# Attention over channels and two gated MLPs on one core: the head rearranged (first loads on two queues, seven split segments, sums of squares folded in PSUM, another TensorE order)

## What is computed

```python
qn = q / (norm(q, axis=1) + 1e-6)          # q, k, v: (1, 6016, 256)
kn = k / (norm(k, axis=1) + 1e-6)
a = softmax(kn.transpose(0, 2, 1) @ qn / tau, axis=-1)   # 256 x 256
x = (v @ a).reshape(6016, 256)
x = (silu(x @ w_gate) * (x @ w_val)) @ w_out             # 256 -> 1536 -> 256
h = x @ w_in                                             # 256 -> 2048
out = (h * clip(h + 3, 0, 6) / 6) @ w_out2               # -> 256
```

## Time and profile before

| | |
|---|---|
| median of 3 runs (lowest, highest) | 1163.73 us (1163.48, 1164.4) |
| the profiled execution: its time, its span | 1163.87 us, 1162.0 us |
| TensorE busy | 1151.7 us, 99% of the span |
| TensorE granted clock, mean | 0.999 |
| VectorE, ScalarE, GpSimd busy | 61%, 23%, 6% |
| first matmul of the main loop; its second | 67.73 us; 68.56 us |

### The profile page before, as it was taken

How to read it: one execution, slowest core, us unless ns; L and a number is a source line. 1 busy time by engine, 2 the same in 40 slices (tenths; PEclk the granted TensorE clock), 3 DMA queues, 4 the chain that set the end, 5 groups by cost and what they waited for, 6 DMA issues and landing times.

```text
span 1162.0 us, 14581 instructions
## 1 busy us (share of the span) xinstructions
PE 1151.7 (99%) x5212; PEld 967.1 (83%) x5212; DVE 711.5 (61%) x1160; ACT 271.8 (23%) x447; POOL 69.7 (6%) x40
## 2 busy tenths in 40 slices
PE   8999999999999999999999999999999999999998
PEld 7878888888888888888888888888888888888998
DVE  5797764664665574485485476466457557548555
ACT  7731311221221221121121122122122122112121
POOL 5593000000000000000000000000000000000000
PEclk9999999999999999999999999999999999999999
DMA  9642020010002002002002002000100200100100
GB/s 354 234 127 55 1 36 0 0 28 8 0 1 35 0 0 36 0 0 37 0 0 36 0 0 36 0 0 15 21 0 0 36 0 0 32 0 0 19 1 14
DMA packets 108751, 33.76 MB, mean 29 GB/s; under 512 B 98752, under 2 KB 103104, under 8 KB 108736
## 3 DMA queue, kind: packets, MB, share of 16 engines
q1 hardware_dynamic: 106704, 33.10, 11.3%
q10 hardware_dynamic: 2032, 0.46, 0.2%
HBM read 27.39 MB, written 6.16 MB: 29 GB/s over the span
## 4 chain that ended last, share of the span: by engine, by line
PE 96%; DVE 2%; DMA 1%; issue 1%; ACT 0%; SPq 0%; ACTq 0%
PE psum L676 33%; PE psum L699 33%; PE psum L687 22%; PE psum L711 6%; PE psum L584 1%; PE psum L659 1%; DMA qk<-in_k 1%; DVE sq_sum L438 1%; DVE vT L452 0%; DVE sq_sum L444 0%; DVE val_w L511 0%; SPq L252 0%; DVE v_turned L498 0%; PE psum L626 0%; ACT qk_parts L349 0%
## 5 line engine op out<-in xcount | busy, mean ns | idle before, releaser
L699 PE MATMUL psum<-prod,down_w 128*128 128x512 f32 (+1 forms) x1728 | 426.9, 384 | 0.0
L699 PEld LDWEIGHTS psum<-prod,down_w 128*128 128x128 f32 x1728 | 322.6, 188 | 61.7
L687 PE MATMUL psum<-yT,up_w 128*128 128x512 f32 (+1 forms) x1152 | 281.4, 384 | 0.0
L687 PEld LDWEIGHTS psum<-yT,up_w 128*128 128x128 f32 x1152 | 214.9, 188 | 41.3
L540 DVE TENSOR_TENSOR act_out<-psum,act_out 128x512 f32<-128x512 f32 (+1 forms) x144 | 97.9, 680 | 236.3 <-PE psum L676 236.3
L676 PE MATMUL psum<-vT,gate_w 128*128 128x512 f32 (+1 forms) x864 | 215.8, 385 | 0.4 <-DVE vT L452 0.4
L676 PE MATMUL psum<-vT,val_w 128*128 128x512 f32 (+1 forms) x864 | 215.4, 384 | 0.0
L402 ACT ACTIVATE act_out<-psum 128x512 f32<-128x512 f32 (+1 forms) x144 | 85.1, 591 | 471.3 <-PE psum L676 448.3
L676 PEld LDWEIGHTS psum<-vT,gate_w 128*128 128x128 f32 x864 | 161.2, 188 | 32.0 <-DVE vT L452 0.9
L676 PEld LDWEIGHTS psum<-vT,val_w 128*128 128x128 f32 x864 | 161.3, 188 | 30.9
L553 DVE SCALAR_TENSOR_TENSOR act_out<-act_out,psum 128x512 f32<-128x512 f32 (+1 forms) x192 | 129.2, 673 | 76.6 <-ACT act_out L410 76.5
(11 more groups left out here) (66 smaller groups left out, 310.4 us busy)
## 6 DMA issues: line engine op xcount, KB each, us to landing
v_in<-in_v SPq DMA_DIRECT2D x44, 128.0 KB, 3.3
out<-out_sb SPq DMA_DIRECT2D x44, 128.0 KB, 2.5
qk<-in_q SPq DMA_DIRECT2D x7, 512.0 KB, 9.1
qk<-in_k SPq DMA_DIRECT2D x7, 512.0 KB, 10.2
w_stage<-in_moe_w_out SPq DMA_DIRECT2D x7, 512.0 KB, 3.9
w_stage<-in_moe_w_in SPq DMA_DIRECT2D x4, 512.0 KB, 3.8
qk_more<-in_q SPq DMA_DIRECT2D x3, 512.0 KB, 10.5
qk_more<-in_k SPq DMA_DIRECT2D x3, 512.0 KB, 11.2
```

The costliest lines, as they stand in the source:

```text
L687: end = mm(HID[j % 4][:, 0:n], up2_w[:, part, b, j * P:(j + 1) * P], yT[:, m, b, 0:n], start=(part, m, b) == (0, 0, 0), stop=(part, m, b) ...
L699: end = mm(banks[h][:, 0:n], w[:, part, j, h * P:(h + 1) * P], prod[:, c % 4, m, 0:n], start=j == 0 and (part, m) == PASSES[0], stop=False)
```

## The change

It does the following. The loads of k for segment 0 are issued on ScalarE's queue, with q's on SP's; `tau` is issued after the squares of the first chunks. Segment 0 is no longer split; segments 1 to 7 are (seven in place of six), in four buffers (`parts_early`, `parts_late`). ScalarE casts only q's high part; GpSimd casts k's (512 columns) and makes both low parts. The last full segment's squares are added in halves of 512 columns, and the folds of `sq_sum` read or write PSUM; segment 11's squares have a bank of their own. TensorE takes NORMS after segment 9 h = 0, with the rest of the halves behind it, and two chunks and segment 11 of h = 1 behind `turn_exp(0)`. v's first tile is transposed into PSUM banks 0 and 1 ahead of the folds, its evictions stand at folds 2 and 4. The table load for Silu moves behind fold 6; the casts of up blocks 3 and 4 stand ahead of the first exponential, block 5 behind the second.

```diff
-    SPLIT_SEGS = 6
-    WHOLE_SEGS = 9
-    EARLY_CASTS = 3
+    SPLIT = range(1, 8)
+    HALVED = 9
+    FULL_SEGS = SEGS - 1
+    BUFFERS = 4
+    EARLY_CASTS, MIDDLE_CASTS = 3, 2
...
+            parts_late = sb("parts_late", [P, 2, 2, 2, NARROW * C], fp32r, early)
...
+        SQ_BOTH = psum[:, 4:8, :].rearrange("p (h b) c -> p h (b c)", h=2)
+        SQ_LAST = psum[:, 3, :].rearrange("p (h c) -> p h c", h=2)
+        V_FIRST = [psum[:, c, :] for c in range(KC)]
...
+        TURNED = (2, 4)
+
+        def load(queue, s, x, begin, end, loaded):
+            at = seg_at(s)
+            queue.dma_start(slot(s)[:, x, begin:end], (q_seg, k_seg)[x][:, at + begin:at + end]).then_inc(loaded, 16)
...
+        def parts(s):
+            n = SPLIT.index(s) % BUFFERS
+            return parts_early[:, n] if n < 2 else parts_late[:, n - 2]
...
-            def load(s, begin, end, loaded):
-                at = seg_at(s)
-                sp.dma_start(slot(s)[:, 0, begin:end], q_seg[:, at + begin:at + end]).then_inc(loaded, 16)
-                sp.dma_start(slot(s)[:, 1, begin:end], k_seg[:, at + begin:at + end]).then_inc(loaded, 16)
-
-            load(0, 0, WIDE * C, seg_loaded[0])
-            load(0, WIDE * C, SEG * C, narrow_loaded)
-            for s in range(1, SLOTS):
-                load(s, 0, SEG * C, seg_loaded[s])
-            for s in range(SLOTS, SEGS):
-
-                sp.wait_ge(seg_multiplied, s - SLOTS + 1)
-                sp.wait_ge(seg_low, min(s - SLOTS + 1, SPLIT_SEGS))
-                sp.wait_ge(squared, 2 * (s - SLOTS + 1))
-                load(s, 0, seg_chunks(s) * C, seg_loaded[s])
+            load(sp, 0, 0, 0, WIDE * C, seg_loaded[0])
+            load(sp, 0, 0, WIDE * C, SEG * C, rest_loaded)
+
+            for s in range(1, SEGS):
+                if s >= SLOTS:
+
+                    sp.wait_ge(seg_multiplied, s - SLOTS + 1)
+                    if s - SLOTS in SPLIT:
+                        sp.wait_ge(q_high, SPLIT.index(s - SLOTS) + 1)
+                        sp.wait_ge(seg_low, SPLIT.index(s - SLOTS) + 1)
+                    sp.wait_ge(squared, 2 * (s - SLOTS + 1))
+                for x in range(2):
+                    load(sp, s, x, 0, seg_chunks(s) * C, seg_loaded[s])
...
-            for s in range(SPLIT_SEGS):
-                pool.wait_ge(seg_high, s + 1)
-                nc.gpsimd.tensor_tensor(qk_parts[:, s % 2, 1], narrow(s), qk_parts[:, s % 2, 0].bitcast(fp32),
+            for i, s in enumerate(SPLIT):
+                pool.wait_ge(seg_loaded[s], 32)
+                if i >= BUFFERS:
+                    pool.wait_ge(parts_used, i - BUFFERS + 1)
+                nc.gpsimd.tensor_copy(parts(s)[:, 0, 1], narrow(s)[:, 1]).then_inc(k_high, 1)
+                pool.wait_ge(k_high, i + 1)
+                pool.wait_ge(q_high, i + 1)
+                nc.gpsimd.tensor_tensor(parts(s)[:, 1], narrow(s), parts(s)[:, 0].bitcast(fp32),
                                         ALU.subtract).then_inc(seg_low, 1)
...
-            act.dma_start(tau_sb[:, :], tau.to_broadcast([P, 1])).then_inc(tau_loaded, 16)
+            load(act, 0, 1, 0, WIDE * C, seg_loaded[0])
+            load(act, 0, 1, WIDE * C, SEG * C, rest_loaded)
...
+            act.dma_start(tau_sb[:, :], tau.to_broadcast([P, 1])).then_inc(tau_loaded, 16)
+
+            for s in range(FULL_SEGS):
                 act.wait_ge(seg_loaded[s], 32)
                 if s == 0:
-                    act.wait_ge(narrow_loaded, 32)
-                if s < SPLIT_SEGS:
-                    if s >= 2:
-                        act.wait_ge(parts_used, s - 1)
-                    nc.scalar.copy(qk_parts[:, s % 2, 0], narrow(s)).then_inc(seg_high, 1)
+                    act.wait_ge(rest_loaded, 32)
+                if s in SPLIT:
+                    i = SPLIT.index(s)
+                    if i >= BUFFERS:
+                        act.wait_ge(parts_used, i - BUFFERS + 1)
+                    nc.scalar.copy(parts(s)[:, 0, 0], narrow(s)[:, 0]).then_inc(q_high, 1)
                 for h in range(2):
                     if s >= 1:
                         act.wait_ge(squares_added, 2 * (s - 1) + h + 1)
-                    nc.scalar.activation(SQ[h][:, 0:width], slot(s)[:, h, 0:width], ACT.Square).then_inc(squared, 1)
+                    nc.scalar.activation(SQ[h], slot(s)[:, h, :], ACT.Square).then_inc(squared, 1)
+            act.wait_ge(seg_loaded[FULL_SEGS], 32)
+            nc.scalar.activation(SQ_LAST, slot(FULL_SEGS)[:, :, 0:LAST_CHUNKS * C], ACT.Square).then_inc(squared, 1)
...
-            cast_up(EARLY_CASTS)
+            for i in range(EARLY_CASTS, EARLY_CASTS + MIDDLE_CASTS):
+                cast_up(i)
 
             def vT_evict(n, c):
-                act.wait_ge(v_read, n * KC + (c + 1))
-                nc.scalar.copy(vT[:, 0, c, :], v_turned[:, c, :]).then_inc(vT_high, 1)
+                act.wait_ge(v_read, c + 1 if n is None else n * KC + (c + 1))
+                turned = V_FIRST[c] if n is None else v_turned[:, c, :]
+                nc.scalar.copy(vT[:, 0, c, :], turned).then_inc(vT_high, 1)
...
-            cast_up(EARLY_CASTS + 1)
             expT_evict(0)
             exponent(1)
-            cast_up(EARLY_CASTS + 2)
-            table_of(ACT.Silu)
...
-                if r in (6, 8):
-                    vT_evict(0, (6, 8).index(r))
+                if r == 6:
+                    table_of(ACT.Silu)
+                if r in TURNED:
+                    vT_evict(None, TURNED.index(r))
...
-            added = 2 * (SEGS - 1)
-            for width in (2 * C, C):
-                dve.wait_ge(squares_added, added)
-                nc.vector.tensor_tensor(sq_sum[:, :, 0:width], sq_sum[:, :, 0:width], sq_sum[:, :, width:2 * width],
+            added = 2 * (FULL_SEGS - 1)
+            half = 2 * C
+            for h in range(2):
+                dve.wait_ge(squared, 2 * (FULL_SEGS - 1) + h + 1)
+                dve.wait_ge(squares_added, 2 * (FULL_SEGS - 2) + h + 1)
+                nc.vector.tensor_tensor(sq_sum[:, h, 0:half], SQ[h][:, 0:half], sq_sum[:, h, 0:half],
                                         ALU.add).then_inc(squares_added, 1)
-                added += 1
+                nc.vector.tensor_tensor(SQ[h][:, half:], SQ[h][:, half:], sq_sum[:, h, half:],
+                                        ALU.add).then_inc(squares_added, 1)
+            added += 4
             dve.wait_ge(squares_added, added)
-            dve.wait_ge(squared, 2 * SEGS)
-            nc.vector.tensor_tensor(sq_sum[:, :, 0:C], SQ_LAST, sq_sum[:, :, 0:C], ALU.add).then_inc(squares_added, 1)
+            nc.vector.tensor_tensor(sq_sum[:, :, 0:C], SQ_BOTH[:, :, half:half + C], sq_sum[:, :, 0:C],
+                                    ALU.add).then_inc(squares_added, 1)
+            nc.vector.tensor_tensor(SQ_BOTH[:, :, half + C:], SQ_BOTH[:, :, half + C:], sq_sum[:, :, C:half],
+                                    ALU.add).then_inc(squares_added, 1)
+            added += 2
+            dve.wait_ge(squares_added, added)
+            nc.vector.tensor_tensor(sq_sum[:, :, 0:C], SQ_BOTH[:, :, half + C:], sq_sum[:, :, 0:C],
+                                    ALU.add).then_inc(squares_added, 1)
+            added += 1
+            dve.wait_ge(squares_added, added)
+            dve.wait_ge(squared, 2 * FULL_SEGS + 1)
+            nc.vector.tensor_tensor(sq_sum[:, :, 0:C], SQ_LAST, sq_sum[:, :, 0:C],
+                                    ALU.add).then_inc(squares_added, 1)
...
+            for c in range(KC):
+                turn_v(None, c)
...
-                if r in (5, 7):
-                    turn_v(0, (5, 7).index(r))
-                if r in (6, 8):
-                    vT_evict(0, (6, 8).index(r))
+                if r in TURNED:
+                    vT_evict(None, TURNED.index(r))
...
+            wide(0, range(WIDE), range(KC))
+            pe.wait_ge(rest_loaded, 32)
+            wide(0, range(WIDE, SEG), range(KC)).then_inc(seg_multiplied, 1)
+
+            for s in SPLIT:
                 wide(s, range(WIDE), range(KC)).then_inc(seg_multiplied, 1)
-                if s >= 1:
+                if s - 1 in SPLIT:
                     split_part(s - 1)
-            split_part(SPLIT_SEGS - 1)
-            for s in range(SPLIT_SEGS, WHOLE_SEGS):
+            split_part(SPLIT[-1])
+            for s in range(SPLIT.stop, HALVED):
                 wide(s, range(SEG), range(KC))
 
-            for s in range(WHOLE_SEGS, SEGS - 1):
-                wide(s, range(SEG), (0,))
-            pe.wait_ge(squares_added, 2 * (SEGS - 1) + 3)
+
+            wide(HALVED, range(SEG), (0,))
+            pe.wait_ge(squares_added, 2 * (FULL_SEGS - 1) + 8)
             for x in range(2 * KC):
                 end = mm(NORMS[:, x:x + 1], sq_sum[:, x // KC, x % KC * P:(x % KC + 1) * P], ones[:, 0:1],
                          start=True, stop=True)
             end.then_inc(norms_summed, 1)
-            wide(SEGS - 1, range(LAST_CHUNKS), (0,), stop=True).then_inc(scores_summed, 1)
```

(44 more changed lines are left out.)

7 lines of the change are left out of this document (2 added, 5 removed).

## The result

| | before | changed |
|---|---|---|
| median of 13 runs (lowest, highest) | 1164.12 us (1163.48, 1165.21) | 1161.04 us (1160.53, 1166.24) |
| ratio to before, 95% interval | | 0.9978 (0.9969 to 0.9987) |
| profiled execution: time, span | 1163.87, 1162.0 us | 1161.04, 1159.2 us |
| NORMS begins; first fold; second matmul of the main loop | 43.86; 51.02; 68.56 us | 41.43; 48.95; 65.98 us |

The kernel is about 0.2% faster, 2.8 us in the profiled executions, and 2.58 of them stand in the head. From the second matmul of the main loop to the end of the span it is 1093.44 us before and 1093.22 after.

The account below looks back on a forecast made before the run. TensorE is busy 99%, so only the head can give: VectorE's sums decide NORMS. The fold's start gains 1.6 us and vT 0.6, 2.2 in all: 1163.87 to 1161.65, less 0.14 is 1161.5 us; range 1162.3 to 1159.5.

Parts of the forecast that it names:

- The total: Whole kernel: 2.2 us gained in the head, 1.6 by the fold's start and 0.6 by vT, giving 1161.5 us.
- The sums decide: Ahead of NORMS: VectorE's sums end at 41.55 us, TensorE arrives at 39.8 and waits 1.75; loads set the pace.
- rival (b): VectorE's first add waits for late tau; landing at 15 to 17.5 costs 1 to 4 us; chance 0.12 with (d).
- The loads: First loads, 3.5 to 7.0 us: tau causes the 2.05 us loss; issuing it later gains the stream 0.3 us.
- Four buffers: Split segments: casts no longer wait for TensorE's buffers, which spread segments over 3.16 us; adds come every 2.375 to 2.48.
- The tail of the sums: VectorE behind segment 10's add: four half adds and the folds take 5.45 us where it was 5.09.
- From NORMS to the folds: TensorE, NORMS to first fold: 14 matmuls instead of 10, 7.8 us where it was 7.16, no bubble left.
- vT: Start of the main loop: turning v ahead of the folds removes the wait for vT, 0.60 us.
- The covers: Folds: Silu table load, second exponential and casts cost nothing, with over 4 us of cover; about 1 us if it failed.
- Rival (d), the clock: TensorE's clock falls in the wait before NORMS; each microsecond of matmuls would cost one more; chance 0.12 with (b).

Follow-up runs that it names:

- the late wait for tau: Changed kernel with VectorE's wait for tau and its one multiply moved from ahead of the first add to behind the last fold: 1161.04 us, ratio 0.9979.
- the changed kernel's second profile: The changed kernel itself timed again, nothing changed, on one chip with two other runs: median 1160.95 us, ratio 0.9972; the profiled execution took 1162.19 us.

## Why the prediction was right, point by point

**The total.** 1161.5 forecast, 1161.04 measured; second matmul of the loop at 66.34 and at 65.98. The head gained 2.58 us where the sum had 2.22: 0.17 more by the sums, 0.28 more behind NORMS, 0.09 less at vT.

**The sums decide: right in size, wrong in what paces them.** Folds done at 41.55 forecast, 41.38 measured; segment 10 added from 36.1 and from 36.10. But I had the loads set the pace from segment 6 on and took tau's landing as a rival (b), harmless up to 11.8. Issued at 4.68 and not at 5.5, and 6.99 us on its way and not 5.9, it landed at 11.66, so this mechanism was already the bound, 0.3 us ahead of the loads, as the late wait for tau and the changed kernel's second profile show. The number came out because both bounds lie at the same place; for this step that is luck.

**The loads: the step that failed.** "I take tau to be the cause" of the slow stretch gave tau all of the 2.05 us. It costs 0.7 to 1.1 of them, and only when its packets run in the first stretch (158 to 204 GB/s in the three profiles where they do); without them the stretch has 284 to 310 GB/s in three profiles with one queue, and 222 to 293 in the seven with two. What is slow in it without tau stays open. The 0.3 us that I took for the stream as a whole was about right, and for the reason given, that the loss comes later: between 3.5 and 14 us the mean rate is 336 GB/s before, 348 with tau alone moved and 351 in the changed kernel, worth 0.3 and 0.4 us.

But the segments did not land 0.3 us sooner: segment 2 began at 14.59, not at 13.9, and TensorE came to NORMS at 40.4, not at 39.8. k's second queue, to which I gave no effect, may have a part in it: in the kernels made from the changed one segment 2 begins at 13.87 and 13.96 in the two profiles with one queue, and at 14.18 to 15.20 in the seven with two and tau behind the squares. Why is not shown, and in the kernel before, with one queue and tau late, its k landed at 15.1 too. Neither cost a thing, since the sums came at 41.4.

**Four buffers:** right; with two of them NORMS is 3.15 us later.

**The tail of the sums:** 5.45 forecast for the adds and folds, 5.28 measured. PSUM matters: without it 2.03 us of contention, and then 1.7 of the clock.

**From NORMS to the folds:** 7.8 forecast, 7.52 measured. The 14 matmuls took 5.94 us where 6.05 was forecast, and no turn-over came on top; no bubble, as forecast. **vT:** 0.60 forecast, 0.51 in the changed kernel and 0.58 alone. **The covers** (Silu table, casts, second exponential) held: no wait in the folds.

**Rival (d), the clock,** cost nothing in the profiled execution, whose wait is 0.99 us, and in most others; in three of 13 the mean clock says that it fell somewhere. I gave a longer wait no price of its own: the three runs that made the wait ahead of NORMS 2.9 us or more paid 1.7 to 2.6 us beside the wait itself.

## What to carry to other kernels

When two chains meet at one point, write down when each arrives and by what it is paced, the smallest load among them too: 0.5 KB that one instruction waits for was the bound here, and its wait belongs where the value is used. Then fill the wait of the engine that decides with its own later work, two matmuls here, before making the other chain faster. And keep two-operand SBUF instructions of VectorE off the chain when GpSimd begins to work beside it.
